# A wide product of ones behind each attention step of the first batch, in a recurrent attention and two feed-forward layers

## The reference

```
f = sigmoid(f_logit)
for t in range(S):                                  # S = 768
    state = f[t] * state + outer(k[t], v[t])        # per batch and head, 48 x 48
    y[t] = q[t] @ state
x = y, heads side by side                           # (4, 768, 384)
u = x + (x^T @ U @ V)^T                             # mixes tokens, rank 32
x2 = u + relu(u @ w_ch1) @ w_ch2                    # 384 -> 1536 -> 384
h = relu(x2 @ w_in)                                 # 384 -> 1024
out = (h * sigmoid(conv3(h, conv_w))) @ w_out       # conv over tokens, 3 taps
```

## Time and profile before

| | us |
|---|---|
| median of 3 runs | 736.3 (735.75 to 736.71) |
| the profiled execution, its own time | 736.56 |
| its span in the trace | 734.8 |
| TensorE busy, matmul | 699.3 (95%) |
| TensorE busy, weight loads | 657.7 (90%) |
| VectorE busy | 446.1 (61%) |
| ScalarE busy | 246.3 (34%) |
| POOL busy | 286.3 (39%) |

### The profile page before, as it was taken

How to read it: one execution, slowest core, us unless ns; L and a number is a source line. 1 busy time by engine, 2 the same in 40 slices (tenths; PEclk the granted TensorE clock), 3 DMA queues, 4 the chain that set the end, 5 groups by cost and what they waited for, 6 DMA issues and landing times.

```text
span 734.8 us, 22489 instructions
## 1 busy us (share of the span) xinstructions
PE 699.3 (95%) x10076; PEld 657.7 (90%) x10076; DVE 446.1 (61%) x709; ACT 246.3 (34%) x504; POOL 286.3 (39%) x262
## 2 busy tenths in 40 slices
PE   2888799999999999999999999999999999999998
PEld 1777599989999889999999989999999889999997
DVE  6994565582798565365598755364489832121875
ACT  1134524333246432212245531313134542121453
POOL 5852567592363135043253224145145311030432
PEclk9999979999999999999999999999999999999999
DMA  8332353421101110200201200120000000000000
GB/s 202 102 89 52 82 141 106 118 73 47 43 1 55 45 54 7 62 24 24 67 2 27 72 34 24 25 65 23 24 2 2 34 33 1 0 1 1 1 33 32
DMA packets 24288, 33.67 MB, mean 46 GB/s; under 512 B 5152, under 2 KB 17184, under 8 KB 24192
## 3 DMA queue, kind: packets, MB, share of 16 engines
q1 hardware_dynamic: 23184, 30.46, 15.2%
q10 hardware_dynamic: 1008, 1.77, 1.1%
HBM read 27.50 MB, written 4.72 MB: 44 GB/s over the span
## 4 chain that ended last, share of the span: by engine, by line
PE 69%; DVE 21%; issue 5%; ACT 3%; DMA 1%; POOL 1%; ACTq 0%; DVEq 0%; POOLq 0%
PE acc L719 8%; PE hb L700 7%; PE acc L720 7%; PE acc L724 6%; PE hb L701 6%; PE hb L702 6%; PE att L585 5%; DVE conv L1112 5%; DVE q_t L1040 4%; PE att L631 3%; DVE conv L1109 3%; PE hb L668 2%; PE acc L758 2%; DVE conv L1096 2%; PE acc L759 2%
## 5 line engine op out<-in xcount | busy, mean ns | idle before, releaser
L1082 DVE SCALAR_TENSOR_TENSOR r_lo<-hb,r_hi 128x386 fp32r<-128x386 f32 (+1 forms) x96 | 53.4, 556 | 185.5 <-ACT r_hi L883 185.5
L883 ACT ACTIVATE r_hi<-hb 128x386 fp32r<-128x386 f32 (+1 forms) x96 | 47.2, 491 | 258.1 <-PE hb L702 258.1
L1200 POOL TENSOR_TENSOR r_lo<-conv,r_hi 128x384 fp32r<-128x384 f32 x64 | 61.8, 965 | 169.2 <-ACT r_hi L898 169.2
L1163 POOL TENSOR_TENSOR k_t<-k_t,blocks 112x512 f32<-112x512 f32 x60 | 82.5, 1376 | 83.3 <-PE att L585 72.3
L719 PE MATMUL acc<-r_hi,w_ch_hi 128*128 128x386 f32 (+1 forms) x288 | 103.7, 360 | 0.0
L700 PE MATMUL hb<-u_hi,w_ch_hi 128*128 128x386 f32 (+1 forms) x288 | 98.8, 343 | 3.0 <-DVE r_lo L1082 2.9
L701 PE MATMUL hb<-u_hi,w_ch_lo 128*128 128x386 f32 (+1 forms) x288 | 98.2, 341 | 0.0
L720 PE MATMUL acc<-r_hi,w_ch_lo 128*128 128x386 f32 (+1 forms) x288 | 97.9, 340 | 0.0
L702 PE MATMUL hb<-u_lo,w_ch_hi 128*128 128x386 f32 (+1 forms) x288 | 97.6, 339 | 0.0
L1112 DVE SCALAR_TENSOR_TENSOR conv<-hb,convw,conv 128x384 f32<-128x384 f32 x128 | 79.1, 618 | 4.5
L585 PEld LDWEIGHTS att<-q_t,k_t 48*64 48x64 f32 (+3 forms) x3840 | 60.0, 135 | 24.2 <-issue 17.6
(11 more groups left out here) (138 smaller groups left out, 1313.5 us busy)
## 6 DMA issues: line engine op xcount, KB each, us to landing
v_p<-in_vn_dram SPq DMA_DIRECT2D x12, 384.0 KB, 3.9
out_dram<-ostage SPq DMA_DIRECT2D x24, 192.0 KB, 2.1
q_t<-in_qT_dram SPq DMA_DIRECT2D x21, 192.0 KB, 3.4
k_t<-in_kT_dram SPq DMA_DIRECT2D x21, 192.0 KB, 3.3
gates<-in_fT_dram SPq DMA_DIRECT2D x21, 192.0 KB, 3.5
ostage<-in_w_ch_dram SPq DMA_DIRECT2D x14, 192.0 KB, 3.3
conv<-in_w_ch_dram SPq DMA_DIRECT2D x10, 192.0 KB, 3.0
ostage<-in_w_out_dram SPq DMA_DIRECT2D x5, 192.0 KB, 2.8
```

Source lines behind the costliest of these rows:

```text
L1163: nc.gpsimd.tensor_tensor(view, view, block_product(ends, c, 1), ALU.mult).then_inc(k_ready, 1)
```

## The change

Behind each TensorE step of the first batch's attention, from level 0 up to the state updates, stands one more fp32 product: `ones` (now 128 x 128) as weights and as the moving operand, read four times over so that 512 columns move, into the third acc bank, which is free then. It waits for nothing, signals nothing and nothing reads it. The first feed-forward product into that bank starts with start=True and overwrites it. L567 takes the first 64 columns of the wider tile.

```diff
-        ones = sb("ones", [P, C])
+        ones = sb("ones", [P, P])
...
-                        pe.matmul(banks[o:o + C, par, :].rearrange("p (g x) -> p g x", x=C)[:, :, 0:32], ones[rows, :],
+                        pe.matmul(banks[o:o + C, par, :].rearrange("p (g x) -> p g x", x=C)[:, :, 0:32], ones[rows, 0:C],
...
+            def busy():
+
+                wide = ones[:].rearrange("p (o t) -> p o t", o=1).broadcast_to([P, 512 // P, P])
+                pe.matmul(acc[:, 2, :].rearrange("p (o t) -> p o t", t=P), ones[:], wide, start=True, stop=True,
+                          skip_group_check=True)
+
...
                 if kind == "att":
                     attention(*task[1:])
+                    if task[1] < DUOS and EVEN < task[2] < Y:
+                        busy()
```

## The result

| | before | changed |
|---|---|---|
| median of the runs, us | 736.02 (735.29 to 736.71, 4 runs) | 752.67 (751.11 to 753.64, 4 runs) |
| the profiled execution, us (span) | 736.56 (734.8) | 752.52 (750.7) |
| last attention product of the first batch ends, us | 76.4 | 92.3 |
| ratio of the times, 95% interval | | 1.0224 (1.0204 to 1.0245) |

The changed kernel is 2.2% slower, by 16.7 us between the medians and 15.9 us between the two spans.

The account below looks back on a forecast made before the run. TensorE, busy 623.85 of 634 us from 101 us on, was taken as the bound; 736.6 + 4.1 for the attention's later end - 0.5 for the stretch behind 92 us gave 740 us, range 732 to 750.

Parts of the forecast that it names:

- What bounds the kernel, and at which clock: TensorE bounds, so the first attention's shift arrives almost whole; it ran at 1.2 GHz from 13 to about 74 us.
- The time as a function of the rise: First batch's attention ends at 71.5 + (W - 18)/2 us if the clock rises at W; break-even at W = 28 us.
- W = 36: Assumed clock rise at 36 us, near duo 2's column sums; attention ends at 80.5, +4.1 us.
- the predicted shift of the attention's end (+4.1): First batch's attention ending at 80.5 instead of 76.4 us.
- two bounds: Small products alone did not raise the clock in 60 us; 2.4 us of wide work behind saturated small work did.
- The late rival: Clock rises only at 32-column steps, transposes and updates, W about 55; attention ends at 90, 750 us; chance 0.28.
- The faster rival: Clock rises at the first column sums, W about 21; attention ends at 73.0, -3.4 us, 733 us; chance 0.32.
- The stretch behind 92 us: Feed-forward's start, 9 us at half clock behind a 2.78 us idle wait; clock's return expected to save 0.5 us.
- That small work does not raise the clock: Small products kept TensorE busy 49.44 of the 59 us to 72 and never raised its clock.
- the rank products: Four wide products (L668) from 71.41 us; some 2.4 us of such work was taken to raise the clock.
- my price from L668: Cost of each added 512-column product on TensorE: 0.86 us at 2.4 GHz, about 1.7 us at 1.2 GHz.

Follow-up runs that it names:

- double: Changed kernel with two products instead of one behind each of the first six steps; 739.9 us, ratio 1.0053.
- burst_double: Changed kernel plus seven products ahead of the first step, two behind the first column sums, and a second behind each of the first six steps; 736.0 us, 1.0013.
- hold_wide: Changed kernel plus seven products at the start, two more behind the first column sums, two instead of one behind the first level; 733.5 to 754.2 us, median 739.8.
- burst_only: Kernel before plus six wide products ahead of the first step, none behind the steps; 734.9 us, ratio 0.9993.
- gap_only: Kernel before plus three products where TensorE waits for r_lo, behind the next batch's first level; 734.4 us, ratio 0.9988.
- early_only: Changed kernel with only the first 12 of the 24 products; 752.2 us, ratio 1.023.
- burst_all: Changed kernel plus six wide products ahead of the first step; 753.0 us, ratio 1.0236.
- late_only: Changed kernel with only the 13 of 24 products from duo 0's last level on; 739.9 us, ratio 1.0051.

## Why the prediction was wrong

- **What bounds the kernel, and at which clock: right.** The whole shift of the attention's end, 15.9 us, arrived at the end of the span (15.9). The reading that the records miss the first, slow stretch is confirmed by the changed trace: steps shorten from 1.9 to 1.14 us at the very time of its first record.
- **The time as a function of the rise: right.** 71.5 + (W - 18)/2, where W is the time of the rise, gives 91.95 with W = 58.9; measured 92.3. That it comes so close is in part luck. Two terms in it were off against each other: a product costs 1.05 us warm and 2.00 cold where I had 0.91 and 1.8 (24 x 0.14 is 3.4 us too little), and the waits that remain are 1.5 us where I left 3.5.
- **The step that failed: W = 36.** I took the place around duo 2's column sums, 33 to 37 us, as dense enough. TensorE was there on time (L567 at 37.30), the products and steps followed each other as densely as planned, and the clock did not rise; nor at 18 to 22 us. It rose around the product behind the first 32-column level, at 58.9, 59.2 and 60.4, in the three kernels with single products from the start, which are alike from the first step up to there. At 0.5 us for each us of delay this is 11.5 of the 11.8 us by which the predicted shift of the attention's end (+4.1) missed the measured one (+15.9). The prediction names two bounds, small work that does not raise the clock and wide work that does, and no row puts the rise at 36 us between them. The late rival (no rise until the 32-column steps, transposes and updates, 750 us) had almost the time. I gave it 0.28, and ended the range 2.7 us short of the result because I took in only half of it. Why the clock rises where it does stays open: double shows that closer wide work brings the rise forward, but not what counts in the alternation with single products.
- **The faster rival** was wrong for this dose, but right as a mechanism: laid in pairs the products raise the clock at 18.4 us (double), or ahead of the steps at 6.5 us. Its price, an end at 71.5 us for 24 products at the full clock, is not refuted. burst_double has six products more than that behind the steps; without them, at 0.98 us each, its 76.1 would be 70.2, plus what they filled of waits (an estimate). But 24 single products do not have the clock to begin with, and where they were given it (hold_wide) they did not hold it in every execution.
- **The stretch behind 92 us** moved along whole: idle 2.78 us again and 10.2 us at half (106.7 to 116.9; before 90.9 to 101.1). The 0.5 us that I took off for it were not there.
- **That small work does not raise the clock** was too strong: in three executions it did with no wide product near, at 54.9 us inside transposes (burst_only) and at 60.4 and 76.2 us in outputs behind a state update (gap_only, early_only). So it is not certain either that the rank products caused the rise at 73.8 us before.

## What to carry to other kernels

Filler work that is to lift TensorE's clock costs about twice as much while the clock is still low (2.00 us against 1.05 here), so price it at the low clock until the trace shows the rise, and lay it close together, where the engine is idle anyway if it can be, rather than as a single product behind every step. Then ask what holds the clock: once the engine is fast it catches up with its suppliers, the other engines and here, it seems, the loading of its own instructions, and what is saved in work comes back as waits. Even so, no version here was faster than the kernel without filler. A break-even as thin as this one (25 us of filler for some 8 us of waits and half of the small work) is worth forecasting as a range over the time of the rise, with the range's end at the latest rise and not halfway to it.

## What the runs showed that I had not expected

- In the changed kernel and the two that are alike from the first step up to there (early_only, burst_all), the same dose raised the clock behind neither the column sums nor any of the eleven steps with 48 to 64 weight columns, and around the first step with 32 columns in all three (58.9, 59.2, 60.4 us). But that is no rule of the 32-column step: in hold_wide the same step, at 53.9 us, passed without a rise, and there as in late_only the clock rose only behind or in the product behind the first transposes (67.5, 53.5 us).
- One kernel can have times 21 us apart (hold_wide, 733.5 to 754.2), and they go with the mean granted clock. In the one that was traced, the longest, the clock was lost behind a pause of 1.3 us at 20 us. With doubled products behind six steps (burst_double) the spread is 6 us.
- A pause that the profile gives to no engine ended 1.2 to 1.6 us behind the landing of a 16 KB packet on the instruction queue in all 36 cases, so such pauses can be looked up there.
- A wide product of 512 columns costs 1.05 us warm and 2.00 cold behind small ones, where my price from L668 was 0.86 and 1.7. In a row of three it costs 0.95 (gap_only, 86.97 to 89.83).
